# Decays moved behind the transposes and the diagonal split between two engines in the recurrent attention of a three-stage kernel

## What is computed

```python
for t in range(S):
    kt, vt, rt = (k[:, :, t], v[:, :, t], r[:, :, t])
    cur = np.einsum('bhd,bhe->bhde', u[None] * kt, vt)
    y[:, :, t] = np.einsum('bhd,bhde->bhe', rt, state + cur)
    state = w[None, :, :, None] * state + np.einsum('bhd,bhe->bhde', kt, vt)
```

## Time and profile before

| | us |
|---|---|
| three runs, median (lowest to highest) | 434.01 (432.62 to 434.83) |
| the profiled execution, its own time | 435.53 |
| its span from first to last instruction | 433.5 |
| first scores on TensorE | 16.62 |
| transposes of unit 4, 5, 6 begin | 36.12, 44.39, 50.70 |
| scores of unit 11 end | 82.93 |
| routing of the first layer begins (VectorE, L845) | 90.18 |
| busy over the span: PE, DVE, ACT, POOL | 379.6, 158.0, 141.9, 173.9 |

### The profile page before, as it was taken

The page is one execution under the profiler, slowest core; times in us unless marked ns, Lnnn a source line. Parts: engine busy times, 40 slices in busy tenths (PEclk is TensorE's granted clock), DMA queues, the critical chain, the costliest instruction groups (busy, mean ns, idle before and its releaser), DMA issues.

```text
span 433.5 us, 10573 instructions
## 1 busy us (share of the span) xinstructions
PE 379.6 (88%) x3300; PEld 358.4 (83%) x3301; DVE 158.0 (36%) x329; ACT 141.9 (33%) x255; POOL 173.9 (40%) x304
## 2 busy tenths in 40 slices
PE   1798899927999999999999999805999999999991
PEld 1597799817999999999999999604999999999990
DVE  4375566685443211111110114038321445415410
ACT  1365455400455222222221125200422454425410
POOL 5884999623302322222222221215242444324511
PEclk9999999976999999999999999956899999999996
...
GB/s 129 136 311 313 206 150 95 54 18 96 391 393 242 21 37 37 37 37 37 37 37 37 37 182 0 42 11 39 352 161 172 342 320 334 165 309 182 27 37 15
DMA packets 66507, 60.40 MB, mean 139 GB/s; under 512 B 43894, under 2 KB 59429, under 8 KB 66481
## 3 DMA queue, kind: packets, MB, share of 16 engines
...
...
## 4 chain that ended last, share of the span: by engine, by line
PE 70%; POOL 9%; issue 7%; DVE 6%; DMA 4%; ACT 1%; POOLq 0%; SPq 0%; DVEq 0%; ACTq 0%
PE p_h L1135 34%; PE p_o L1164 27%; POOL sc L525 4%; PE p_sm L1116 2%; PE p_xt L1104 2%; POOL prod L512 2%; DMA xg<-x_rows,src_idx 2%; DMA x_rows<-y_row,dst_now 1%; POOL r_sc L507 1%; PE p_yt L1110 1%; DMA w_col<-in_w 1%; DMA lg<-x_rows 1%; DVE row_oh L345 1%; DVE k_sc L765 1%; PE p_sm L1120 1%
## 5 line engine op out<-in xcount | busy, mean ns | idle before, releaser
L1135 PE MATMUL p_h<-xT,w_sb 128*128 128x128 f32 x1296 | 152.5, 279 | 1.4 <-ACT xT L622 1.4
L1135 PEld LDWEIGHTS p_h<-xT,w_sb 128*128 128x128 f32 x1296 | 151.6, 195 | 1.9 <-issue 1.9
L948 DVE SCALAR_TENSOR_TENSOR h_lo<-p_h,h_hi 128x512 fp32r<-128x512 f32 x54 | 37.4, 692 | 162.4 <-ACT h_hi L707 162.4
L1164 PE MATMUL p_o<-w_hi,h_hi 128*128 x216 | 76.8, 356 | 0.0
L1164 PE MATMUL p_o<-w_lo,h_hi 128*128 x216 | 74.6, 345 | 0.0
L1164 PE MATMUL p_o<-w_hi,h_lo 128*128 x216 | 73.0, 338 | 0.0
L707 ACT ACTIVATE h_hi<-p_h 128x512 fp32r<-128x512 f32 x54 | 32.3, 598 | 114.5 <-PE p_h L1135 114.5
L537 POOL TENSOR_TENSOR dst_mark<-zeros 128x1 f32<-128x1 f32 x54 | 13.6, 252 | 137.8 <-DVE y_row L960 102.5
L797 DVE TENSOR_TENSOR w_lo<-w_raw,w_hi 128x1024 fp32r<-128x1024 f32 x36 | 42.1, 1221 | 14.6 <-ACT w_hi L622 14.5
L1164 PEld LDWEIGHTS p_o<-w_hi,h_hi 128*128 128x128 f32 x216 | 40.6, 188 | 3.1 <-issue 3.1
L1164 PEld LDWEIGHTS p_o<-w_lo,h_hi 128*128 128x128 f32 x216 | 40.7, 188 | 0.3
...
...
## 6 DMA issues: line engine op xcount, KB each, us to landing
...
xg<-x_rows,src_now POOLq DMA_INDIRECT x27, 3.7
```

The source lines that it names most:

```text
L948: stt(h_lo[:, at, :], p_h[n][:, :, :], 0.0, h_hi[:, at, :].bitcast(F32), ALU.max, ALU.subtract).then_inc(h_ready[layer], 1)
L1135: last = mm(p_h[half][:, f, :], w1_sb[place][:, c, col:col + P], xT[:, c, :], start=(c == 0), stop=(c == DC - 1))
L1164: last = mm(p_o[:, 0:DM], lhs[:, f, :], rhs[:, here], start=(f == 0 and m == 0), stop=(f == FC - 1 and m == 2))
```

## The change

- k and r are transposed as they were loaded. Their buffers get 64 columns a head, of which the last 16 are set to zero once (by VectorE for k; by GpSimd for r, ahead of the memset that signals `ones_set`). VectorE takes both transposes out of PSUM, multiplying by the decay powers `pk` and `pr` on the way (`turned`). ScalarE's three copies, `scale_r` and `r_tab` are gone.
- k times its table, still needed for the state, moves from VectorE to GpSimd, and is made for unit n in unit n.
- GpSimd writes the diagonal of the even heads only (512 elements); ScalarE writes that of the odd heads, with four instructions of 128 columns whose scale is a column of `bonus` (`diagonal`), first in its unit.
- rT keeps both heads of a pair in one tile. The product of state and r takes 64 partitions to 64 (a quarter of TensorE's array each), where before it took 112 to 64; its output and that of v times sc go to a bank each for even and odd heads, and ScalarE copies them out with two instructions instead of one.
- Powers are made up to T/2 only, the last one being squared for the state's decay; only one table is turned, after the first transposes. Some waits in `values` are dropped.

```diff
--- before.py
+++ after.py
-            pw = sa("pw", [P, HP, T + 1])
+            pw = sa("pw", [P, HP, T // 2 + 1])
+            decay = sa("decay", [P, HP])
...
-            r_tab = sa("r_tab", [P, HP, 2, HD])
-            k_tab = sa("k_tab", [P, HP, 2, HD])
+            k_tab = sa("k_tab", [P, H, HD])
             u_tab = sa("u_tab", [P, H, D])
 
 
-            k_raw = [sa(f"k_raw{q}", [P, H, D]) for q in range(RING)]
+            k_raw = [sa(f"k_raw{q}", [P, H, HD]) for q in range(RING)]
             v_raw = [sa(f"v_raw{q}", [P, H * D + HD - D]) for q in range(RING)]
-            r_raw = [sa(f"r_raw{q}", [P, H, D]) for q in range(RING)]
-            k_sc = [sa(f"k_sc{b}", [P, HP, 2, HD]) for b in range(B)]
-            r_sc = [sa(f"r_sc{b}", [P, HP, 2, HD]) for b in range(B)]
+            r_raw = [sa(f"r_raw{q}", [P, H, HD]) for q in range(RING)]
+            k_sc = [sa(f"k_sc{b}", [P, H, HD]) for b in range(B)]
             kT = sa("kT", [P, HP, T])
-            rT = [sa(f"rT{b}", [P, 2, HP, T]) for b in range(B)]
+            rT = [sa(f"rT{b}", [P, HP, T]) for b in range(B)]
...
-            p_y = pb("p_y", [P, HP, T])
+            p_y = pb("p_y", [P, 2, HP, T])
...
-                    sp.wait_ge(r_scaled, n + 1)
+                    sp.wait_ge(kr_turned, n + 1)
...
             gp.memset(w_col[:, :], 1.0)
+            for t in r_raw:
+                last = gp.memset(t[:, :, D:HD], 0.0)
+            last.then_inc(pads_clear, 1)
             gp.memset(eye_wg1[:, :, :], 0.0).then_inc(ones_set, 1)
...
-            def scale_r(i, q, n, b):
-
+            def unit(i, q, n, b, c):
                 pool.wait_ge(raw_loaded[q], 48 * (i + 1))
-                wait_pos(pool, kr_turned, n - 1)
-                gp.tensor_tensor(r_sc[b][:, :, :, 0:D], by_head(r_raw[q]), r_tab[:, :, :, 0:D], ALU.mult)\
-                    .then_inc(r_scaled, 1)
-
-            def unit(i, q, n, b, c):
                 wait_pos(pool, bonus_sum, n)
-                gp.tensor_tensor(prod1[:, :, :], r_raw[q][:, :, :], u_tab[:, :, :], ALU.mult).then_inc(bonus_prod, 1)
+                gp.tensor_tensor(prod1[:, :, :], r_raw[q][:, :, 0:D], u_tab[:, :, :], ALU.mult).then_inc(bonus_prod, 1)
                 pool.wait_ge(bonus_prod, 2 * n + 1)
-                gp.tensor_tensor(prod2[:, :, :], prod1[:, :, :], k_raw[q][:, :, :], ALU.mult).then_inc(bonus_prod, 1)
-                if q < RING - 1:
-                    scale_r(i, q + 1, n + 1, 1 - b)
-                else:
-                    if isinstance(i, int):
-                        scale_r(i + 1, 0, n + 1, 1 - b)
-                    else:
-                        with pool.If(i < NU // RING - 1):
-                            scale_r(i + 1, 0, n + 1, 1 - b)
+                gp.tensor_tensor(prod2[:, :, :], prod1[:, :, :], k_raw[q][:, :, 0:D], ALU.mult).then_inc(bonus_prod, 1)
+                if isinstance(n, int) and n == 0:
+                    pool.wait_ge(tables_ready, 1)
+                wait_pos(pool, kv_made, n - 1)
+                gp.tensor_tensor(k_sc[b][:, :, 0:D], k_raw[q][:, :, 0:D], k_tab[:, :, 0:D], ALU.mult).then_inc(k_scaled, 1)
                 pool.wait_ge(bonus_sum, n + 1)
                 wait_pos(pool, y_made, n - 1)
-                gp.tensor_tensor(sc[b][:, :, :, :], ident[:, :].unsqueeze(1).unsqueeze(2).broadcast_to([P, 2, HP, T]),
-                                 bonus[:, :].rearrange("p (g j) -> p j g", j=2).unsqueeze(3).broadcast_to([P, 2, HP, T]),
+                gp.tensor_tensor(sc[b][:, 0, :, :], ident[:, :].unsqueeze(1).broadcast_to([P, HP, T]),
+                                 bonus[:, :].rearrange("p (g j) -> p j g", j=2)[:, 0, :].unsqueeze(2).broadcast_to([P, HP, T]),
                                  ALU.mult).then_inc(bonus_diag, 1)
...
-            for n, (tab, p_t) in enumerate(((k_tab, p_kt), (r_tab, p_rt))):
-                act.wait_ge(powers_turned, n + 1)
-                copy(tab[:, :, :, :].rearrange("p g j d -> p g (j d)")[:, :, 0:R], p_t[:, :, 0:R]).then_inc(tables_ready, 1)
-            act.wait_ge(cleared, 3)
+            act.wait_ge(powers_turned, 1)
+            copy(k_tab[:, :, :].rearrange("p (g j) d -> p g (j d)", j=2)[:, :, 0:R], p_x[:, :, 0:R]).then_inc(tables_ready, 1)
+            act.wait_ge(consts, 1)
...
-                copy(yT[0:R, :, :], p_y[0:R, :, :]).then_inc(yT_ready, 1)
-
-            def unit(i, q, n, b, c):
-                act.wait_ge(kr_turned, n + 1)
-                wait_pos(act, scored, n)
-                copy(kT[0:R, :, :], p_kt[0:R, :, :]).then_inc(kT_ready, 1)
-                wait_pos(act, y_made, n - 1)
                 for j in range(2):
                     at = slice(HD * j, HD * j + D)
-                    last = copy(rT[b][at, j, :, :], p_rt[at, :, :])
-                last.then_inc(rT_ready, 1)
+                    last = copy(yT[at, :, :], p_y[at, j, :, :])
+                last.then_inc(yT_ready, 1)
+
+            def diagonal(n, b):
+
+                act.wait_ge(bonus_sum, n + 1)
+                wait_pos(act, y_made, n - 1)
+                for g in range(HP):
+                    last = sa.activation(sc[b][:, 1, g, :], ident[:, :], ACT.Copy, scale=bonus[:, 2 * g + 1:2 * g + 2])
+                last.then_inc(bonus_diag, 1)
+
+            def unit(i, q, n, b, c):
+                diagonal(n, b)
...
+            def turned(n, b):
+
+                dve.wait_ge(kr_turned, n + 1)
+                wait_pos(dve, scored, n)
+                tt(kT[0:R, :, :], p_kt[0:R, :, :], pk[0:R, :, :], ALU.mult).then_inc(kT_ready, 1)
+                wait_pos(dve, y_made, n - 1)
+                tt(rT[b][0:R, :, :], p_rt[0:R, :, :], pr[0:R, :, :], ALU.mult).then_inc(rT_ready, 1)
...
-                wait_pos(dve, bonus_diag, n)
+                wait_pos(dve, bonus_diag, 2 * n)
...
-                dve.wait_ge(bonus_diag, n + 1)
+                dve.wait_ge(bonus_diag, 2 * n + 2)
...
+                turned(n, b)
                 bonus_of(n)
-                if q < RING - 1:
-                    scale_k(i, q + 1, n + 1, 1 - b)
-                else:
-                    if isinstance(i, int):
-                        scale_k(i + 1, 0, n + 1, 1 - b)
-                    else:
-                        with dve.If(i < NU // RING - 1):
-                            scale_k(i + 1, 0, n + 1, 1 - b)
...
+            def turn_kr(i, q, n):
+
+                pe.wait_ge(raw_loaded[q], 48 * (i + 1))
                 wait_pos(pe, kT_ready, n)
                 for g in range(HP):
-                    turn(p_kt[0:R, g, :], two(k_sc[b], g), ident[:, :])
-                pe.wait_ge(r_scaled, n + 1)
+                    turn(p_kt[0:R, g, :], two(k_raw[q], g), ident[:, :])
                 wait_pos(pe, rT_ready, n)
                 for g in range(HP):
-                    last = turn(p_rt[0:R, g, :], two(r_sc[b], g), ident[:, :])
+                    last = turn(p_rt[0:R, g, :], two(r_raw[q], g), ident[:, :])
                 last.then_inc(kr_turned, 1)
...
-                        last = mm(p_kv[rows_of(j), g, :], k_sc[b][:, g, j, :], heads(v_raw[q])[:, 2 * g + j, :],
+                        last = mm(p_kv[rows_of(j), g, :], k_sc[b][:, 2 * g + j, :], heads(v_raw[q])[:, 2 * g + j, :],
...
-                pe.wait_ge(rT_ready, n + 1)
-                wait_pos(pe, state_ready, 2 * n - 2)
-                wait_pos(pe, yT_ready, n)
+                if isinstance(n, int) and n == NU - 1:
+                    pe.wait_ge(state_ready, 2 * n - 2)
                 for g in range(HP):
                     for j in range(2):
-                        mm(p_y[rows_of(j), g, :], st[b][0:R, g, :], rT[b][0:R, j, g, :],
+                        mm(p_y[rows_of(j), j, g, :], st[b][rows_of(j), g, :], rT[b][rows_of(j), g, :],
                            start=(g == 0), stop=False, skip_group_check=True)
                 pe.wait_ge(masked, n + 1)
                 for g in range(HP):
                     for j in range(2):
                         h = 2 * g + j
-                        last = mm(p_y[rows_of(j), g, :], v_raw[q][:, h * D:h * D + HD], sc[b][:, j, g, :],
+                        last = mm(p_y[rows_of(j), j, g, :], v_raw[q][:, h * D:h * D + HD], sc[b][:, j, g, :],
                                   start=False, stop=(g == HP - 1), skip_group_check=True)
...
-                        last = mm(p_sc[:, j, g, :], kT[at, g, :], rT[b][at, j, g, :], start=True, stop=True)
+                        last = mm(p_sc[:, j, g, :], kT[at, g, :], rT[b][at, g, :], start=True, stop=True)
...
-                turn_kr(n, b)
+                turn_kr(i, q, n)
+                if isinstance(n, int) and n == 0:
+                    turn_powers()
```

65 lines of the change are left out of this document (29 added, 36 removed).

## The result

The changed kernel takes 439.34 us (median of 4, 438.07 to 440.87) where the kernel before took 433.31 (median of 4, three of them the runs of the table ahead): ratio 1.0155, 95% interval 1.0115 to 1.0194, slower by 6.0 us. It lies above the range that I gave. Its profiled execution took 439.30, with a span of 437.6.

A forecast was written before the change was run, and what follows sets the result against it. TensorE's 5.36 us a unit was taken as the bound, GpSimd no longer late. Unit 5 -0.55, units 6 to 10 +2.45, end +0.7, start 0 gave +2.6 us: forecast 436.5 us, range 433.0 to 438.4.

The forecast's parts named there:

- three signs of being wrong: Unit 5's transposes beginning before 43 us, gaps around the quarters missing, or TensorE's `rows` never waiting.
- The start: Units before 5: first scores several us sooner, but covered by ScalarE's wait for the matrix landing at 26.2; costed at 0.
- unit 5: Unit 5 would begin at 44.4 and last 5.76 us for 6.31, a gain of 0.55.
- The sum: Unit 5 -0.55, units 6 to 10 +2.45, end +0.7, start 0: together +2.6 us.
- Rival 2: Unit 5's loads land ahead of the zeros, units 5 and 6 start up to 1.8 sooner: +0.8, 434.8 us; chance 0.12.
- The quarters: State times r on TensorE: two more changes of shape at 0.2 us each, 0.4 a unit, making it 5.76.
- Rival 3: Quarters run closer together, the state-times-r block of 0.82 could halve to 0.41: 432.7 us, at best 431.5; chance 0.08.
- The loop: TensorE's `rows` waits on ScalarE's output copy behind diagonal and bonus sum: 5.66 or 5.95 a unit, 5.85 taken.
- The end: Unit 11 to routing: `rows(10)` waits for the loop, 13.2 or 13.8 us for 12.68; +0.7 taken.
- Rival 4: Start's gain comes through, unit 4's loads issued some 4 us sooner and landing sooner: 432.6 to 431.6 us; chance 0.08.

The follow-up runs named there:

- e2: Kernel before with the state-times-r product on quarters and the three waits ahead of it dropped: 434.2 us, ratio 1.0014.
- e14: Kernel before with the zeros' store behind all units and the matrix splits behind first exponentials and routing, repeated in more rounds: 429.8 us, ratio 0.9900.
- e15: Kernel before with only the three waits ahead of the state-times-r product dropped: 432.58 us, ratio 1.0007.
- e16: Kernel before, unchanged, profiled a second time: 433.36 us for the profiled execution.
- e3: Changed kernel with ScalarE's copies of the rows ahead of its diagonal writes: 436.33 us, ratio 1.0112.
- e4: Changed kernel with ScalarE's three matrix splits, and VectorE's first two, all in unit 3: 438.32 us, ratio 1.0126.
- e1: Kernel before with the buffers of k and r at 64 columns a head instead of 48: 434.55 us, ratio 1.0052.
- e7: Changed kernel with zeros' store behind all units, splits behind first exponentials and routing, r's pads zeroed behind `ones_set`: 435.73 us, ratio 1.0060.
- e12: Changed kernel with zeros, splits and r's pads late, ScalarE's rows ahead of its diagonal, matrices issued behind all units' loads: 429.76 us, ratio 0.9925.
- e13: Kernel before with zeros and splits late and the matrices issued behind the loads of all units: 429.01 us, ratio 0.9885.
- e6: Kernel before with the zeros' store behind all units and the splits behind the first exponentials and first routing: 429.08 us, ratio 0.9900.
- e11: Kernel before with zeros and splits late and the matrices issued behind unit 7's loads: 434.01 us, ratio 1.0015.
- e9: Changed kernel with zeros, splits and r's pads late and the matrices issued behind unit 7's loads: 438.11 us, ratio 1.0113.
- e10: Changed kernel with zeros, splits and pads late, matrices behind unit 7's loads, ScalarE's rows ahead of its diagonal: 431.89 us, ratio 0.9969.
- e8: Changed kernel, zeros, splits, pads late; state product on 112 rows with a second r eviction, output in one copy, rows before diagonal: 432.83 us, ratio 1.0011.
- e5: Kernel before with the bulk store of the zeros issued behind ScalarE's work of all twelve units: 431.59 us, ratio 0.9972.

## Why the prediction was wrong

**The direction was right, the size was not**: +2.6 forecast, +4.6 at the routing in the trace, +6.0 in the medians. Unit 6 began at 51.56, outside the 50 +- 0.5 forecast; none of the three signs of being wrong that I had named came.

*The step that failed is "The start. ... I cost this at nothing".* Its cover was "a matrix that lands at 26.2 whatever the attention does". It does depend on it. With the old pitch (before, e2, e14, e15, e16) the matrix is issued at 16.4 to 17.4 and lands at 23.9 to 26.2, so that even there 26.2 is only the late end; in the changed kernel, e3 and e4 it is issued at 19.65 to 19.80 and lands at 28.2 to 28.8. The loads' new pitch accounts for 1.0 to 2.1 us of the issue (e1). The pads ahead of `ones_set` delay the first load by 0.56 (2.88 for 2.32), but not the matrix, since e7, which has them later, still issues it at 19.59. Some 1 us more in the changed kernel's first loads stays open, and so does why the matrix lands at 28 and more, since with the pitch alone (e1) it landed at 25.65. The queue behind the matrix had been made longer by the change: diagonal and two output copies stand behind `split_high`, and four us of TensorE's wait and 1.6 of low clock came of it (e4, without that queue, begins unit 4 at 35.16, not 39.14). I had named that queue and then taken "from 26.2 as before" for all that hangs on it. Both had a part: by an estimate from the rows, with the matrix 2.6 us sooner the same queue would still have held `rows(1)` until 30.2, for 1.6 us, and unit 3 would have ended at 35.0, as unit 4's v landed (35.1). In unit 5 what I had left out is VectorE's own split (1.22 us, at 40.74), which pushed the evictions, the bonus sum and ScalarE's copies back, so that `rows(3)` waited 1.12: 6.78 and not 5.76. Without the splits there (e7) unit 5 lasts 5.64. Start and unit 5 together missed by 0.39 + 1.02 = 1.4 of the 2.0 in the trace; the other 0.6 is the end.

*The sum was made against one outcome of a race.* Unit 5's late load looked like a fixture of the kernel before ("units 4 and 5 wait for their loads"), e16 shows that it isn't. Beside e16 the changed kernel's traced execution is 5.9 us longer (439.30 for 433.36), close to the medians' 6.0, and reaches the routing 8.3 later: 4.2 by the start of unit 5, 1.4 in unit 5, 1.5 in units 6 to 10, 1.2 behind. Against that outcome the start, costed at nothing, is the largest term. Rival 2 described the mechanism rightly, and it even came true (unit 5's v landed at 39.5, zeros issued at 38.18), but only after the late matrix had eaten the gain.

*The quarters.* Right in kind: gaps beside the block, none of them hidden. The term was 0.40 and is 0.28 (e2, e15): 0.14 ahead of the block, 0.20 behind it, and 0.07 less for v times sc. The Trainium skill ("TensorEngine Tiling (Array Packing)", Key Properties) says that a change of tiling mode drains the engine; the runs agree in that two more changes cost 0.28. Rival 3 did not come: the block's 16 loads take 0.85 where they took 0.86, and 1.02 from start to start where it was 0.82. The Trainium skill (same page, Performance Considerations, Row Tiling) has 2x row tiling for a contract dimension of 64; the runs show no gain from it here.

*The loop.* Right, and nearly to the number: 5.85 for units 6 to 10. VectorE's multiplying evictions take 0.68, diagonal writes 0.39, both as forecast; the decay takes 0.335 to 1.173, 0.865 in the mean over units 6 to 10, so it is held up there:

```profile
L758 DVE TENSOR_TENSOR kT<-p_kt,pk x12: 676/679/692, 12.1 to 83.2; 112x512 f32<-112x512 f32 x12
...
L760 DVE TENSOR_TENSOR rT<-p_rt,pr x12: 673/676/681, 12.7 to 83.8; 112x512 f32<-112x512 f32 x12
...
L654 ACT ACTIVATE sc<-ident,bonus x48: 384/386/405, 14.0 to 85.9; 128x128 f32<-128x128 f32 x48
...
L778 DVE TENSOR_TENSOR st<-st_sum,decay x11: 335/628/1173, 23.4 to 88.1; 128x192 f32<-128x192 f32 x11
```

I was partly lucky: TensorE's own unit is 5.64, not 5.76, and the loop comes in from unit 8 on only, at 6.0, not 5.95. e3 takes most of it away.

*The end.* +1.32 for 0.7: `rows(10)` waits 1.31 where it didn't wait, and `rows(11)` 1.53 where 0.94 was, as the output is copied in two. With the splits behind the routing it is more: 1.60 in e12 beside e13, 3.2 in e7 beside e6. Before, a split of the matrix on VectorE stood ahead of the last logits, which then waited for nothing:

```profile
87.39 1.23 DVE L797 TENSOR_TENSOR w_lo<-w_raw,w_hi 128x1024 fp32r<-128x1024 f32 x1
...
89.68 0.25 DVE L965 TENSOR_REDUCE lg_sum<-lg_parts 128x16 f32<-128x64 f32 x1
```

In the changed kernel the split (90.61) is over in time, and the last logits wait 1.30 for ScalarE. I had 13.8 as the upper end of that stage; it took 14.00.

*Rival 4* (the start comes through) was rightly held unlikely, and for the reason given: in e7 the 3 MB of matrices stand before unit 4's loads. With them out of the way (e12 beside e13) the first unit begins 2.70 us sooner and unit 4 still 2.08 (32.84 for 34.92).

## What to carry to other kernels

When a change makes a stage early, follow every queue to the next thing that does not move with it, and ask what the change has added behind that thing; a wait of some us there can cost more than its length, as the clock fell behind five of the nine waits listed below. Where two transfers are issued within a few us of each other, look at more than one execution before a sum rests on who was first. Look for the transfer that nobody needs yet: moving the zeros and the splits away gave 1.0% (e6, e14), where the change, with its early start and its lighter GpSimd, gained nothing in any pair.

## What the runs showed of the chip

- Behind waits of 2.50 us (e11), 3.00 (e4), 3.21 (e9), 4.23 (changed kernel) and 5.08 (e1) TensorE was granted 0.50 to 0.55 of its clock for the next 3.7 to 5.2 us, and the unit that followed or was under way took 1.6 to 2.9 us more on top of the wait. Behind waits of 2.07 (kernel before), 2.21 (e10), 2.25 (e8) and 2.41 (e7) the clock stayed at 1.00.
- A store of 2.3 MB issued ahead of the end of SP's issue of a 192 KB load moved that load's landing from 35.7 to 43.8; with the issue over 0.1 to 3.3 us ahead of the store (e15, e16, e2) the load landed at 35.7 to 36.5. The next unit's loads pay then: v of unit 6 landed at 45.3 in e16, and at 40.0 without the store (e5).
- What follows the routing's start, the same work in all kernels but for the splits that e6 to e14 have there, took 340.8 to 345.3 us (span less the routing's start). It went with the clock granted around the second routing, over the same 25 us, counted from 200 us behind the first routing: in the eight traces at 0.71 to 0.74 it took 343.3 to 345.3, in the ten at 0.76 to 0.81 it took 340.8 to 343.1. Three of them, e16 (345.0), the kernel before (343.3) and e12 (341.4):

```profile
286.46:311.46 25.00, 16.67 (x156) 16.16 (x157) 15.40 (x65) 4.79 (x8) 8.48 (x13) 0.71 0.47 160
```

```profile
290.18:315.18 25.00, 17.94 (x159) 17.43 (x156) 15.89 (x59) 5.40 (x8) 9.95 (x14) 0.74 0.53 183
```

```profile
285.61:310.61 25.00, 18.03 (x168) 17.44 (x166) 16.29 (x59) 5.72 (x8) 11.63 (x18) 0.81 0.55 189
```

This is why e5 gained 4.6 us up to the routing and 2.6 over the span (its stretch behind took 345.3), and why traces of single executions are compared here up to the routing. Whether the clock sets the time or goes with it, and what sets it from run to run, stays open.
